# Fused attention and two MLPs: the last tile's layer 2 taken apart between the first steps of stage 2, tile 1's product moved, loops unrolled, opening and tail reordered

## The reference

```python
k_p = k.reshape(B, H, S // 8, 8, D).mean(axis=3)
v_p = v.reshape(B, H, S // 8, 8, D).mean(axis=3)
attn = softmax(q @ k_p.transpose(0, 1, 3, 2) / sqrt(D))
x = (attn @ v_p).transpose(0, 2, 1, 3).reshape(4608, 512)
h = maximum(maximum(x @ w1, x @ w2), x @ w3)     # 512 -> 768
x2 = h @ moe_w_out                               # 768 -> 512
h2 = x2 @ w_in                                   # 512 -> 2048
out = (h2 - tanh(h2)) @ moe2_w_out               # 2048 -> 512
```

## Time and profile before

| | |
|---|---|
| median of 3 runs | 1463.26 us |
| the profiled execution | 1463.32 us |
| its span, first to last instruction | 1461.6 us |
| TensorE busy, mean granted clock | 1432.7 us, 0.993 |
| VectorE busy | 1019.4 us |
| ScalarE busy | 642.4 us |
| GpSimd busy | 94.6 us |
| HBM read and written | 210.89 and 57.15 MB |

### The profile page before, as it was taken

One profiled execution on the slowest core, in us unless ns is written; L12 is line 12 of the kernel. 1 busy time (PEld: TensorE's weight loads), 2 busy tenths in 40 slices (PEclk: granted clock), 3 DMA queues, 4 the chain that ended last, 5 costly groups with the idle time before them and its releaser, 6 DMA issues.

```text
span 1461.6 us, 27906 instructions
## 1 busy us (share of the span) xinstructions
PE 1432.7 (98%) x10776; PEld 1240.2 (85%) x10776; DVE 1019.4 (70%) x1781; ACT 642.4 (44%) x1275; POOL 94.6 (6%) x140
## 2 busy tenths in 40 slices
PE   8999999999999999998899999999999999999998
PEld 7978888888887878787799898899998999999997
DVE  7866666666666646534788778787877878787776
ACT  4322222222222222223566565665655565665654
POOL 2402121212121100000000000000000000000000
PEclk9999999999999999999999999999999999999999
DMA  9234444444443220236867667676766767676551
GB/s 341 80 118 170 159 152 162 141 164 142 162 145 126 93 101 9 101 144 256 299 206 257 223 226 241 209 253 207 250 224 215 246 215 253 208 251 223 192 179 45
DMA packets 78765, 269.97 MB, mean 185 GB/s; under 512 B 6880, under 2 KB 21216, under 8 KB 66976
## 3 DMA queue, kind: packets, MB, share of 16 engines
q1 hardware_dynamic: 78624, 268.07, 52.8%
HBM read 210.89 MB, written 57.15 MB: 183 GB/s over the span
## 4 chain that ended last, share of the span: by engine, by line
PE 94%; DMA 2%; DVE 2%; issue 1%; ACT 1%; SPq 0%; ACTq 0%; DVEq 0%
PE psum L620 30%; PE psum L671 27%; PE psum L696 25%; PE psum L634 9%; PE psum L563 2%; PE psum L603 2%; DMA x_scratch<-x_stage 1%; DMA ring<-w_scratch 1%; DMA v_first<-in_v 0%; PE psum L641 0%; DVE probs L978 0%; DMA k_raw<-in_k 0%; DMA k_first<-in_k 0%; DVE x_stage L1041 0%; PE psum L582 0%
## 5 line engine op out<-in xcount | busy, mean ns | idle before, releaser
L620 PE MATMUL psum<-x,w 128*128 128x512 f32 (+1 forms) x2160 | 453.1, 370 | 5.2 <-DVE x L989 4.3
L671 PE MATMUL psum<-w_out_s,g 128*128 128x512 f32 x1728 | 445.5, 393 | 1.6 <-DVE g L1069 1.6
L620 PEld LDWEIGHTS psum<-x,w 128*128 128x128 f32 x2160 | 376.5, 189 | 76.3 <-issue 6.2
L671 PEld LDWEIGHTS psum<-w_out_s,g 128*128 128x128 f32 x1728 | 306.6, 189 | 53.0 <-DVE g L1069 2.4
L696 PEld LDWEIGHTS psum<-x_even,ring 128*128 128x128 f32 x1680 | 225.7, 194 | 25.3 <-ACT copies L850 6.4
L696 PE MATMUL psum<-x_even,ring 128*128 128x256 f32 x1680 | 230.5, 286 | 11.6 <-DMA ring<-w_scratch 6.1
L1076 DVE SCALAR_TENSOR_TENSOR poly<-poly,u_sq 128x512 f32<-128x512 f32 x144 | 99.5, 691 | 162.1 <-ACT poly L847 162.1
L696 PEld LDWEIGHTS psum<-x_odd,ring 128*128 128x128 f32 x1344 | 178.0, 191 | 13.6 <-ACT h L858 1.9
L696 PE MATMUL psum<-x_odd,ring 128*128 128x256 f32 x1344 | 181.4, 283 | 2.3 <-ACT h L858 1.4
L850 ACT ACTIVATE copies<-psum 128x256 f32<-128x256 f32 x288 | 101.1, 376 | 170.7 <-PE psum L696 170.7
L782 ACT ACTIVATE h<-best 128x512 fp32r<-128x512 f32 (+1 forms) x60 | 35.3, 589 | 268.3 <-DVE best L1004 268.3
(11 more groups left out here) (72 smaller groups left out, 975.9 us busy)
## 6 DMA issues: line engine op xcount, KB each, us to landing
ring<-w_scratch SPq DMA_DIRECT2D x72, 1024.0 KB, 5.1
ring<-w_scratch SPq DMA_DIRECT2D x72, 768.0 KB, 4.4
x_scratch<-x_stage SPq DMA_DIRECT2D x18, 1792.0 KB, 6.2
x_odd<-x_scratch SPq DMA_DIRECT2D x28, 512.0 KB, 5.5
x_even<-x_scratch SPq DMA_DIRECT2D x28, 512.0 KB, 5.4
w_scratch<-w_stage SPq DMA_DIRECT2D x32, 384.0 KB, 2.6
v_raw<-in_v SPq DMA_DIRECT2D x21, 512.0 KB, 4.2
q_t<-in_q SPq DMA_DIRECT2D x36, 256.0 KB, 4.2
```

Source lines behind the costliest of these rows:

```text
L620: mm = pe.matmul(psum[:, bank, 0:hi - lo], w123[:, m, ws, n, c, :], x[:, xs, c, lo:hi], start=(c == 0 and ws + xs == 0), stop=(c == KC1 - ...
L671: mm = pe.matmul(psum[:, j, :], g[:, m % 4, gs, j * P:(j + 1) * P], w_out_s[:, m, ws, :], start=(m == 0 and gs + ws == 0), stop=(m == MC2 ...
```

## The change

1. **Last tile's layer 2.** ORDER ends with l2(8, 0), step 0, x2_part(8, 2), step 1, step 2, first_project. Layer 2 of c = 2, 1 and 3 is done in steps 0, 1 and 2, a third of the block's m between the products. The first two chunks are projected after step 2. The intermediate results of steps 0 to 2 lie in tensors of their own (early_g, early_tanh, early_big) over x.
2. **Splits and stores of the last x2** are put into steps 1 to 3 of ScalarE and VectorE; both engines wait for all stores at the start of step 4. SyncE stores half 0 after step 0 and half 1 in step 3, behind the first ring load of that step.
3. **Loads.** The first ring loads follow layer 1 of m = 1 and m = 2 of the last tile, x2_even follows m = 4; the late pieces of w_out follow step 2 of SyncE; they are split in steps 3 to 7 instead of 1 to 5. Tile 1's x2 is loaded in steps 4 to 7.
4. **Tile 0.** attend(2), the product of tile 1, comes behind the second layer-2 block instead of the third.
5. **No loops in stage 2.** All 72 steps are straight code on all engines.
6. **Opening.** SyncE waits for k_first_in[2] instead of k_first_in[0] before q(1); the second warming of 14 is cut into 10 before the pooling of v and 4 behind it; norm is cut in two entries (sums, and turn with scaling and transposes); high(1) comes behind attend(0), high(3) ahead of scores 2 and 3, turn(3) behind high(5).
7. **Tail.** The last step's half 1 is finished ahead of its half 0 (row_of gives chunks 142 and 143 their exchanged rows of w_out).

```diff
@@ make_order
-        ("warm", 14), ("score", 0), ("score", 1), ("pool_v",), ("warm", 14), ("norm", 0), ("high", 0), ("norm", 1),
-        ("high", 1), ("low", 0), ("attend", 0), ("low", 1), ("high", 2)]
+        ("warm", 14), ("score", 0), ("score", 1), ("warm", 10), ("pool_v",), ("warm", 4), ("norm", 0), ("turn", 0),
+        ("high", 0), ("norm", 1), ("turn", 1), ("low", 0), ("attend", 0), ("high", 1), ("low", 1), ("high", 2)]
...
+    then(("l2", NT - 1, C_ORDER[0]), ("step", 0), ("x2_part", NT - 1, C_ORDER[1]), ("step", 1),
+         ("step", 2), ("first_project",))
@@ SyncE
-            sp.wait_ge(k_first_in[0], 16)
+            sp.wait_ge(k_first_in[2], 16)
...
+            def step(s):
+                t, p = s // STEPS2, s % STEPS2
+                if 0 < t < NT - 1 and p < PRODUCTS:
+                    load_x2(t + 1, p)
+                if t > 0 and p == 2:
+                    store_out(t - 1)
+                if s + 2 < ALL2:
+                    sp.wait_ge(multiplied, PRODUCTS * s + 4)
+                    load_w((p + 2) % STEPS2, 0)
+                if s == EARLY:
+                    store_last_x2(1)
+                if t == 0 and p > EARLY:
+                    if p == EARLY + 1:
+                        sp.wait_ge(g_ready, 2 * EARLY)
+                    for n in range(2 * (p - EARLY - 1), min(2 * (p - EARLY), PRODUCTS)):
+                        load_x2(1, n)
+                if s + 2 < ALL2:
+                    sp.wait_ge(multiplied, PRODUCTS * s + PRODUCTS)
+                    load_w((p + 2) % STEPS2, 1)
+            step(0)
+            store_last_x2(0)
+            for s in range(1, EARLY):
+                step(s)
+            wait_filled(sp, ("l2", NT - 1, C_ORDER[-1]))
+            for kind, n in LATE:
+                load_piece(PIECES.index((kind, n)))
@@ TensorE, called where project_before was
+            def between(s, n):
+                if s < EARLY:
+                    if n < 3:
+                        layer2(("l2", NT - 1, C_ORDER[s + 1]), range(2 * n, 2 * n + 2))
+                else:
+                    project(2 * (s - 2) + n // 2, (0, 1) if n % 2 == 0 else (2, 3))
@@ ScalarE, step(s)
+                if s == EARLY + 1:
+                    act.wait_ge(x2_stored, 16 * KHALF * NT)
+                if s > 0:
+                    copy_last(s - 1)
+                    square(s - 1, 0)
+                    shifted_square(c, 0, 0)
...
+                if s == 1:
+                    x2_sums_high(NT - 1, 0)
+                if s == 2:
+                    x2_high(("l2", NT - 1, C_ORDER[2]))
+                if s == EARLY:
+                    x2_sums_high(NT - 1, 1)
@@ ScalarE, behind the last step
+            act.wait_ge(summed, 3 * ALL2)
+            square(s, 1)
+            shifted_square(c, 1, 0)
+            copy_last(s)
+            g_hi(c - 1, 1)
+            tanh(s, 1)
+            square(s, 0)
+            shifted_square(c + 1, 0, 1)
+            tanh(s, 0)
+            g_hi(c, 0)
@@ VectorE, step(s)
+                if s == EARLY + 1:
+                    dve.wait_ge(x2_stored, 16 * KHALF * NT)
...
+                if s == 1:
+                    x2_sums_low(NT - 1, 0)
+                sum_first(s)
+                if s == 2:
+                    x2_sums(("l2", NT - 1, C_ORDER[2]))
+                if s == EARLY:
+                    x2_sums_low(NT - 1, 1)
...
+                sum_second(s)
+                if s == 2:
+                    x2_sums(("l2", NT - 1, C_ORDER[3]))
```

More of the change, by code:

```diff
@@ L48 @@
 STEPS2 = MC2 // 2
+ALL2 = NT * STEPS2
+EARLY = 3
 PRODUCTS = 7
@@ L177 @@
 L1_NUMBER = {e: i for i, e in enumerate(e for e in ORDER if e[0] == "l1")}
-for _kind, _count in (("score", STEPS), ("norm", STEPS), ("attend", len(ATTENDS))):
+for _kind, _count in (("score", STEPS), ("norm", STEPS), ("turn", STEPS), ("attend", len(ATTENDS)), ("step", EARLY)):
     assert [e[1] for e in ORDER if e[0] == _kind] == list(range(_count))
@@ L501, in _ @@
-            with sp.Fori(0, 3) as i:
-                tile(2 * i + 1, 1)
-                tile(2 * i + 2, 0)
-            tile(7, 1)
-            tile(8, 0)
+            step(0)
[5 more added lines that the diff above has]
+                load_piece(PIECES.index((kind, n)))
+            for s in range(EARLY, ALL2):
+                step(s)
+                if s == STEPS2 - 1:
+                    sp.wait_ge(x2_stored, 16 * KHALF * NT)
@@ L728, in tile @@
-            def tile(t, odd):
-                for p in range(STEPS2):
-                    step(t, p, odd)
-            pe.wait_ge(shifted, STEPS)
-            wait_x(pe, len(ATTENDS) - 1)
-            for p in range(2):
-                step(0, p, 0)
-            for bank in range(4):
-                pe.wait_ge(drained[bank], BANK_USES[bank])
-            for p in range(2, STEPS2):
-                step(0, p, 0)
-            with pe.Fori(0, 3) as i:
-                tile(2 * i + 1, 1)
-                tile(2 * i + 2, 0)
@@ L748, in _ @@
+            for s in range(EARLY, ALL2):
+                step(s)
+            for c in range(2 * ALL2 - 4, 2 * ALL2):
+                project(c, range(SUB))
         @block.scalar
@@ L905, in tile @@
-            def tile(t):
-                for p in range(STEPS2):
-                    step(t, p)
-            act.wait_ge(w_stored, 48 * UNITS)
-            tile(0)
-            with act.Fori(0, 3) as i:
-                tile(2 * i + 1)
-                tile(2 * i + 2)
-            tile(7)
-            tile(8)
-            last = MC2 * NT - 1
-            first_of(NT - 1, STEPS2 - 1)
-            tanh(0, STEPS2 - 1)
-            g_hi(last - 2, MC2 - 3)
-            act.wait_ge(summed, 3 * STEPS2 * NT)
@@ L922, in _ @@
-            square(last, 1, STEPS2 - 1)
-            tanh(1, STEPS2 - 1)
-            shifted_square(last, 1)
-            g_hi(last - 1, MC2 - 2)
+                if entry == ("step", 0):
+                    act.wait_ge(w_stored, 48 * UNITS)
+                if entry[0] == "x2_part":
+                    x2_high(("l2",) + entry[1:])
+                if entry[0] == "step":
+                    step(entry[1])
+            for s in range(EARLY, ALL2):
+                step(s)
+            s, c = ALL2 - 1, 2 * ALL2 - 2
```

531 lines of the change are left out of this document (260 added, 271 removed).

## The result

The changed kernel takes 1444.54 us (median of 4, 1443.24 to 1445.42) against 1463.22; the ratio is 0.987 with a 95% interval of 0.9857 to 0.9882, 18.7 us less. I had forecast 1439.4 and a range up to 1444.5: the direction and most places were right, but the gain is 5 us short, and the time lies on the very edge of the range.

The account below looks back on a forecast made before the run. TensorE, busy 98% of the span, was taken as the bound, with its holes and half-clock stretches. Gains of 13.5 (boundary), 2.9, 4.7, 1.7 and 1.1 sum to 23.9 us: 1463.3 to 1439.4 us, range 1434.5 to 1444.5.

Parts of the forecast that it names:

- Boundary, 17.0 us of holes: Between the stages, up to step 3: 17.0 us of holes and half clock go if layer 2 fills between products.
- The margins I took as 0: Steps 0 to 2: loads, ScalarE copies (at most 0.5 a step), banks and store of half 0 (0 to 0.6) cost nothing.
- The wait for the store of half 1: Step 4: TensorE waits 2.3 us behind the store, plus 0.9 for half clock; 3.2 us lost, bounds 0 and 5.2.
- x2 for tile 1: Loads moved to steps 4 to 7, the last behind a ring load in step 7: 0.3 us lost (0 to 1).
- Loops: Stage 2: two loop edges of 1.17 and 1.69 us go, 2.9 us gained; straight code costs 0 (up to 2).
- Tile 0: Passage to tile 1: 3.3 us hole and 1.75 of slow clock go, late bank costs 0.3; gain 4.7 (4 to 5).
- Opening: Start of the kernel: earlier attend 0.8 us, layer 1 without hole and slow matmuls 0.9; gain 1.7 (-0.5 to 2.5).
- Tail: Last projections: holes for g shrink and the end moves from 1458.3 to 1457.1; gain 1.1 us (0.5 to 1.6).
- A: Rival: the store of half 1 lands in time, 3.2 us more go, 1436.2 us; chance 20%.
- B: Rival: ScalarE and VectorE bind the first steps, step 4's wait at its upper bound, opening gains nothing; 1444.6 us; 20%.
- C: Rival: slower, straight code of 48 more steps makes an engine's instruction fetch stall; 1467 us; chance 3%.
- D: Rival: the boundary's 17 us come back as waits for loads, taking nearly all of the 13.5; 1453 us; 4%.

Follow-up runs that it names:

- e10: e1 with the last tile's four layer-2 blocks run in a row, nothing between the products of steps 0 to 2; 1447.43 us.
- e1: Changed kernel with the store of x2's half 1 issued ahead of the 1024 KB ring load in SyncE's step 3; 1438.56 us, ratio 0.9836.
- e3: Changed kernel with ScalarE and VectorE waiting for the x2 stores at the start of step 5 instead of step 4; 1437.9 us, ratio 0.983.
- e2: Changed kernel with eight of the ten late w_out loads moved behind SyncE's step 3; 1444.54 us.
- e8: Kernel before with only its stage 2 loops written out as straight code on four engines; 1461.15 us, ratio 0.9985.
- e4: Changed kernel with 10 warming entries behind the v pooling instead of 4; 1445.2 us.
- e7: e1 with 15 warming entries ahead of the v pooling and 10 behind it; 1442.58 us.
- e12: Changed kernel with the changes of e1 and e3, q(1) gated on k_first_in[0], and 15 and 7 warming entries around the v pooling; 1440.16 us, ratio 0.9837.
- e11: e1 with the old tail: half 0 of the last step ahead of half 1, no exchanged rows; 1439.62 us, ratio 0.983.
- e5: e1 with the whole opening of the kernel before put back; 1439.62 us, ratio 0.984.
- e9: Kernel before with only tile 1's product moved behind tile 0's second layer-2 block instead of the third; 1460.69 us, ratio 0.9977.

## Why the prediction was right, and where it was off

- **Boundary, 17.0 us of holes.** Right: 16.9. The margins I took as 0 (x2_even at 11.0 us, copies behind a piece of 1.38 us, the banks, the store of half 0) all held; there is no hole in steps 0 to 2. e10 shows that taking out the filler alone gives half of it back, a split that I did not forecast.
- **The wait for the store of half 1.** Right in mechanism, place and releaser; its size is the term of the sum that was wrong. The store was issued at 697.68, 4.8 us into step 3 (forecast 4.7). It landed 15.7 us into the step, I had taken 13.3 and 14.4 as the bound. ScalarE then took 3.1 us as forecast. The hole was 4.6 instead of 2.3 us, and with it the full clock cost of 1.7 us instead of the half that I took: 6.3 instead of 3.2, above my bound of 5.2. The failure is the step that reads 2816 KB off rows of loads alone and then takes something off because the store alone is quick: load and store in one queue took 11.2 us from the first issue (257 GB/s). e1 removes the wait by order, e3 by need; e2 excludes the w_out loads.
- The rule that I cited from the page "DMA: Bandwidth & Descriptors" of the Trainium skill, section "Queues, rings and completion order", had the right sign: the increment waits for earlier writes. The traces are in line with it in both orders (second place: 10.9 us for the store, 8.8 for the load; first place: 6.7 and 6.9). They don't single it out: two transfers that are merely served one behind the other would look the same.
- **x2 for tile 1.** Forecast 0.3 us, measured 0.2.
- **Loops.** 2.9 by the trace as forecast; e8 measures 2.2 (0.7 to 3.5). The page "Runtime: NRT & Kernel Launch" of the Trainium skill, section "Instruction fetch mechanics", calls the cost of crossing a block boundary in straight code mostly hidden; in the 68 steps of e8 nothing of it shows. Whether the holes on "issue" in the openings of e4, e7 and e12 are such a cost is not shown. As evidence the 30 steps of the earlier trace rows were weaker than I made them: about half of them lie in the last round of the loop.
- **Tile 0.** Forecast 4.7 us, measured 5.1 at the place; the late bank that I priced at 0.3 cost nothing.
- **Opening.** Wrong: 1.7 forecast, -0.9 in the profile. The step that failed is the one that took full clock for granted once the long hole was broken up. The product did start 0.7 us earlier, and the rest of layer 1, up to the next product at 46.82 us, took 0.4 less (forecast 0.9), but the half-clock stretch that lay under the v pooling and the warming matmuls before now lies under layer 1 and costs 2.4 us. The start of layer 2 of tile 0 in the profiles with exactly the new opening (changed kernel, e1, e2, e3, e10, e11) is 82.27, 81.22, 81.28, 81.40, 80.70, 82.66; with the old one (before, e5, e8, e9) 81.40, 81.51, 81.65, 82.02. The means are 81.6 and 81.6: nothing gained or lost on average. The spread of the new one follows the clock: the first group of layer 1 took 6.96, 6.04, 6.03, 6.05, 4.54 and 7.21 us in the same six. So the changed kernel's profile was a poor draw, and e10's, at 80.70, a good one with full clock throughout:

```profile
17.90 1.56 PE L640 MATMUL psum<-turned,v_pooled 32*64 32x256 f32 x48 [1.41 <-DVE turned L1027]
20.50 4.54 PE L657 MATMUL psum<-x,w 128*128 128x256 f32 x36 [1.04 <-DVE x L1033]
```

- **Tail.** Forecast 1.1 us, measured 1.05 (the two ends that I wrote down, 1458.3 and 1457.1, would give 1.2).
- **Rivals.** A (the store in time, 1436.2) did not happen; e1 and e3, which take the wait away, come to 1438.6 and 1437.9. B came out near in time (1444.6) for another reason: its wait in step 4 and its opening without gain are there, the failing margins of steps 0 to 2 are not, and the wait alone is larger than it said. C and D are excluded: from step 8 on the steps take 10.56 us each, and the boundary is 16.9 us shorter.

What stays open: why stage 1 loses 0.3, 3.1 and 1.6 us to waits for drained banks in e4, e7 and e12, the three kernels with more warming matmuls, and nothing in the changed kernel and e1; what TensorE's holes on "issue" in the same three are; and whether e9's missing 1.3 us are spread or place.

## What to carry to other kernels

Where a whole stage's start waits on one last transfer, look at what the same queue was given just before it: a load that was needed only two steps later, issued 0.4 us ahead of a store that two engines wait for, cost 6 us here, and exchanging the two lines gave them back. Work put between dependent products is worth the holes and the half-clock stretches that it fills (7.9 us here). What moves with it, here the store, needs a check of its own: who waits for it next, and what stands ahead of it. In an opening bound by loads and a softmax chain, more warming matmuls gained nothing here: in e4 they moved the half-clock stretch, and in e7 and e12, where it was gone, other holes came to as much or more.

## What the hardware showed that I had not expected

Behind a hole of 4.6 us the granted clock stood at half until 3.3 us after TensorE resumed (1.7 us lost), and behind the 3.29 us hole of the earlier trace rows it cost 1.75 us. Shorter holes did it too, but not reliably. In the opening of the changed kernel holes of 1.35, 1.69 and 0.99 us were followed by half clock (2.4 us lost). In e10, with the same code there and holes of 1.57, 1.41 and 1.04 us, the clock stayed at 1.00. The single holes of 0.9 and 1.4 us at the loop edges of the kernel before left it at 1.00 as well. So the lengths of the holes alone do not tell here whether the clock falls.

With 12 to 22 more small matmuls in the opening and the DMA engines at a share of 1.00, TensorE stood 1.0 to 1.5 us on "issue" between 29 and 33 us in e4, e7 and e12, which none of the other kernels shows there. I took them for stalls of the instruction fetch; the traces don't show that. A packet of instructions is loaded at 28 to 30.5 us in e4, e7 and e12, and also in e1 and e10, which have no such hole.
